# The second output product of pair 1 made whole at the end of its phase, as that of pair 2 is

## What is computed

```
x   = rms_norm(x) * rms_g
x   = (silu(x @ w_gate) * (x @ w_val)) @ w_out        # FFN 1, 1536 hidden columns
out = silu(x @ w2_in) @ w2_out                        # FFN 2, 2048 hidden columns
```

## Time and profile before

| what | value |
|---|---|
| median of 3 runs | 873.72 us (873.68 to 873.9) |
| the profiled execution, its own time | 873.36 us |
| its span, first to last instruction | 871.6 us |
| PE busy | 862.1 us, 99% |
| DVE busy | 545.3 us, 63% |
| ACT busy | 351.2 us, 40% |
| POOL busy | 413.5 us, 47% |
| DMA | 229.47 MB, mean 263 GB/s |
| granted TensorE clock | 0.5 up to 17.3 us, then 1.0 |

### The profile page before, as it was taken

The page is one execution under the profiler, slowest core; times in us unless marked ns, Lnnn a source line. Parts: engine busy times, 40 slices in busy tenths (PEclk is TensorE's granted clock), DMA queues, the critical chain, the costliest instruction groups (busy, mean ns, idle before and its releaser), DMA issues.

```text
span 871.6 us, 13511 instructions
## 1 busy us (share of the span) xinstructions
PE 862.1 (99%) x5112; PEld 830.8 (95%) x5112; DVE 545.3 (63%) x840; ACT 351.2 (40%) x648; POOL 413.5 (47%) x425
## 2 busy tenths in 40 slices
PE   7999999999999999999999999999999999999998
PEld 7999999999999999999899899999998998999998
DVE  6789757766557666655564355679676754345862
ACT  3679744542222223346553122225334332234531
POOL 6898999882347681657773000130035545203200
PEclk9999999999999999999999999999999999999999
DMA  9971678778899994656779366776768788586671
GB/s 261 280 202 32 250 276 322 276 290 316 303 332 356 348 354 152 242 199 259 267 295 372 151 236 259 275 280 254 298 239 325 266 311 290 200 311 260 242 274 73
DMA packets 79488, 229.47 MB, mean 263 GB/s; under 512 B 22720, under 2 KB 47296, under 8 KB 66752
## 3 DMA queue, kind: packets, MB, share of 16 engines
q1 hardware_dynamic: 79424, 228.61, 72.8%
HBM read 153.09 MB, written 75.50 MB: 262 GB/s over the span
## 4 chain that ended last, share of the span: by engine, by line
PE 97%; DVE 1%; DMA 1%; ACT 0%; issue 0%; SPq 0%; DVEq 0%; ACTq 0%
PE ps L1918 17%; PE ps L1920 16%; PE ps L1919 16%; PE ps L1986 5%; PE ps L1987 5%; PE ps L1985 5%; PE ps L1960 4%; PE ps L1962 4%; PE ps L1961 4%; PE ps L1847 4%; PE ps L1816 2%; PE ps L2051 2%; PE ps L2050 2%; PE ps L2049 2%; PE ps L2015 2%; PE ps L2016 2%
## 5 line engine op out<-in xcount | busy, mean ns | idle before, releaser
L1918 PE MATMUL ps<-xh,wr 128*128 128x384 f32 x840 | 282.7, 337 | 0.1
L1920 PE MATMUL ps<-xh,wr 128*128 128x384 f32 x840 | 281.3, 335 | 0.0
L1919 PE MATMUL ps<-xl,wr 128*128 128x384 f32 x840 | 281.1, 335 | 0.0
L1918 PEld LDWEIGHTS ps<-xh,wr 128*128 128x128 f32 x840 | 157.7, 188 | 3.7 <-DVE qt L1502 1.2
L1919 PEld LDWEIGHTS ps<-xl,wr 128*128 128x128 f32 x840 | 157.7, 188 | 0.6
L1920 PEld LDWEIGHTS ps<-xh,wr 128*128 128x128 f32 x840 | 157.7, 188 | 0.0
L1987 PE MATMUL ps<-wo,al 128*128 128x512 f32 x192 | 75.0, 391 | 0.0
L1986 PE MATMUL ps<-wo,ah 128*128 128x512 f32 x192 | 75.0, 390 | 0.0
L1985 PE MATMUL ps<-wo,ah 128*128 128x512 f32 x192 | 74.7, 389 | 0.0
L1521 DVE TENSOR_TENSOR qt<-ps,qt 128x384 f32<-128x384 f32 x84 | 46.0, 555 | 41.6 <-PE ps L1920 41.4
L1146 ACT ACTIVATE qt<-qt 128x384 f32<-128x384 f32 x102 | 52.5, 523 | 45.8 <-DVE qt L1521 45.3
(11 more groups left out here) (198 smaller groups left out, 1816.5 us busy)
## 6 DMA issues: line engine op xcount, KB each, us to landing
wr<-ring_home SPq DMA_DIRECT2D x40, 1792.0 KB, 8.4
ring_home<-wr SPq DMA_DIRECT2D x20, 1792.0 KB, 8.0
out_home<-wo SPq DMA_DIRECT2D x14, 1024.0 KB, 9.3
wo<-out_home SPq DMA_DIRECT2D x14, 1024.0 KB, 8.0
fw<-fold_home SPq DMA_DIRECT2D x7, 1536.0 KB, 6.7
ending_home<-eb SPq DMA_DIRECT2D x16, 512.0 KB, 6.1
ew<-ending_home SPq DMA_DIRECT2D x4, 2048.0 KB, 7.9
raw_c<-in_moe_w_out SPq DMA_DIRECT2D x13, 512.0 KB, 8.1
```

The costliest lines, as they stand in the source:

```text
L1918: pe.matmul(out_ps, w_hi, x_hi, start=first and c == 0, stop=False, skip_group_check=True)
L1919: pe.matmul(out_ps, w_hi, x_lo, start=False, stop=False, skip_group_check=True)
L1920: ins = pe.matmul(out_ps, w_lo, x_hi, start=False, stop=c == 1, skip_group_check=True)
```

## The change

Phase 4 becomes like phase 5. Its Silu columns are kept in `eh`, it has no downs, and an ending follows its last unit; the eight downs of phase 4 go. The functions of the ending get an argument e, 0 for phase 4 and 1 for phase 5. With it:

- The products of both endings come in a new order, forms 0, 1, 3, 4, 5, 6, 2 of the first factor. Products 0 and 1 share two PSUM banks in turns, so tile 2 of product 1 (i = 1, t = 2) waits for the column sum c11 of tile 0, and DVE's order at the start of an ending is rewritten.
- Low and high parts of product 0 are made in the last two units, two each.
- POOL makes weight sums c0 to c3 in phase 3, ahead of that phase's hidden sums, and c4 to c7 after the whole product; then for each ending four sums of form 3 and four of form 5. The sums have two homes in SBUF.
- Phase 5's token forms are made within the ending of phase 4, from product 3 on. Ring loads of units 52 to 54 wait for that ending (products 4 and 5), and the output of pair 1 is stored behind the ring load of unit 55.
- SP's queue has an `ending` item for each; the weights of an ending come into four homes, with product 0's load asked for at the third last unit.

```diff
-    WHOLE, ENDING = 3, 5
-
-    XHOME = [0, 1, 0, 1, 1, 0]
+    WHOLE, ENDINGS = 3, (4, 5)
+
+    XHOME = [0, 1, 0, 1, 1, 1]
...
-            pending = None if ph in (WHOLE, ENDING) else len(downs)
+            pending = None if ph >= WHOLE else len(downs)
             downs.append((ph, g))
         if ph == WHOLE:
             items.append(("whole", ph))
-    items.append(("ending", ENDING))
+        if ph in ENDINGS:
+            items.append(("ending", ph))
...
+    EPRODUCTS = [(0, 0, 0, True), (0, 1, 1, True), (2, 3, 3, True), (1, 4, 4, True), (1, 5, 5, False), (1, 2, 6, False),
+                 (2, 6, 2, False)]
...
-    ESUMS = {"u2": (0, 1), "u3": (ET, 2), "c22": (ET + 1, 2), "c11": (3 * ET, 1), "c21": (4 * ET, 1),
+    ESUMS = {"c11": (0, 1), "u2": (ET, 1), "u3": (2 * ET, 2), "c22": (2 * ET + 1, 2), "c21": (4 * ET, 1),
              "c12": (5 * ET, 1)}
...
+    EHOME = [0, 1, 2, 0, 1, 3, 0]
+    pieces = [EPART if fw < 3 else 1 for _, fw, _, _ in EPRODUCTS]
+    e_load = [[16 * sum(pieces[m] * (e + (m <= i)) for m in range(NF) if EHOME[m] == EHOME[i]) for i in range(NF)]
+              for e in range(2)]
+
+    ELOW_AT = [[], [], [], [0, 1, 2], [3, 4], [5, 6, 7], [8, 9, 10]]
+    EHIGH_AT = [[], [], [], [0], [1, 2, 3], [4, 5], [6]]
...
+    CHOME = [1, 0, 1, 0, 0, 1, 0, 1]
+    C_AT = {first_unit[(WHOLE, WHOLE + 1)[j // EPART]] + (2, 4, 6, 7, 0, 2, 3, 4)[j]: j for j in range(2 * EPART)}
...
+                if u in ending_next:
+                    sp.wait_ge(s_end, ET * (5 if u == ending_next[0] else 6))
...
+            def load_ending(e, i):
+
+                f, done = EPRODUCTS[i][1], ET * NF * e
+                if i == 0 and e == 0:
+                    sp.wait_ge(s_wh, 2 * NF)
+                    sp.wait_ge(s_cst[1], 32 * EPART)
+                    sp.wait_ge(s_cst[0], 32 * EPART)
+                elif i == 0:
+                    sp.wait_ge(s_end, done)
                 elif i < 3:
-                    sp.wait_ge(s_prod, NF * (last_unit[ENDING] + i - 1))
-                else:
-                    sp.wait_ge(s_end, ET * (i - 2))
+                    sp.wait_ge(s_prod, NF * (last_unit[ENDINGS[e]] + i - 1))
+                elif i == 5:
+
+                    sp.wait_ge(s_elo, EPART * (NF * e + 5))
+                else:
+                    sp.wait_ge(s_end, done + ET * (i - 2))
...
+                if kind == "ending":
+                    for i in range(2, NF):
+                        load_ending(ENDINGS.index(x), i)
+                    if x == ENDINGS[0]:
+                        for u in ending_next:
+                            load_ring(u)
...
-                if item == ("unit", first_unit[WHOLE + 1]):
+                if item == ("down", last_down[WHOLE - 1]):
                     load_raw(made_at["c", 0])
-                if kind == "unit" and 0 < x - first_unit[WHOLE + 1] <= 2 * EPART:
-                    keep(made_at["c", x - first_unit[WHOLE + 1] - 1])
-                if item == ("unit", first_unit[ENDING] + 2):
-                    load_ending(0)
-                if item == ("unit", last_unit[ENDING] - 1):
-                    load_ending(1)
+                if item == ("unit", first_unit[WHOLE] + 1):
+                    load_raw(made_at["c", 1])
+                if item == ("whole", WHOLE):
+                    load_raw(made_at["c", 5])
+                if kind == "unit" and x in C_AT:
+                    keep(made_at["c", C_AT[x]])
+                for e, ph in enumerate(ENDINGS):
+                    if item == ("unit", last_unit[ph] - 2):
+                        load_ending(e, 0)
+                    if item == ("unit", last_unit[ph] - 1):
+                        load_ending(e, 1)
+                if item == ("unit", first_unit[ENDINGS[1]]):
+                    sp.wait_ge(s_ec, esum(0, "c12", ET - 1))
+                    store(ENDINGS[0], range(PT))
...
+            for j in range(EPART):
+                ending_weight_sums(made_at["c", j])
             first_group = downs.index((WHOLE, 0))
             for j in range(PART):
                 hidden_sums(3, j)
             for j in range(PART):
                 hidden_sums(5, j)
-            for i in range(MADE, len(made)):
-                ending_weight_sums(i)
-            for f in (3, 5):
-                for j in range(EPART):
-                    ending_hidden_sums(f, j)
+            pool.wait_ge(s_wh, 2 * NF)
+            for j in range(EPART, 2 * EPART):
+                ending_weight_sums(made_at["c", j])
+            for e in range(2):
+                for f in (3, 5):
+                    for j in range(EPART):
+                        ending_hidden_sums(e, f, j)
...
+            def act_ending(e):
+                u = last_unit[ENDINGS[e]]
+                silu(u, 2)
+                silu(u, 3)
+                ending_high(e, 1, [EPART - 1])
                 for t in range(ET):
-                    ending_copy(t)
-                for i in range(2, NF):
-                    ending_high(i)
+                    ending_copy(e, t)
+                for i in range(1, NF):
+                    if i + 1 < NF:
+                        ending_high(e, i + 1)
+                    if e == 0:
+                        for f in EHIGH_AT[i]:
+                            token_high(ENDINGS[1], f)
...
-                if ph == ENDING and EPART - 1 <= g < 2 * EPART - 1:
-                    ending_high(0, [g - EPART + 1])
-                if x == last_unit[ENDING]:
-                    ending_high(1)
+                if ph in ENDINGS and g >= 2 * EPART - 2:
+                    i = g - 2 * EPART + 2
+                    ending_high(ENDINGS.index(ph), 0, range(2 * i, 2 * i + 2))
+                if ph in ENDINGS and x == last_unit[ph]:
+                    ending_high(ENDINGS.index(ph), 1, range(EPART - 1))
...
+            def dve_ending(e):
+                ending_low(e, 1)
+                ending_low(e, 2, (0, 1))
+                ending_sum(e, "c11", 0)
+                ending_low(e, 2, (2, 3))
+                for j in range(EPART):
+                    ending_hidden_sums(e, 4, j)
+                ending_sum(e, "c11", 1)
+                ending_sum(e, "c11", 2)
+                for i in range(2, NF):
                     if i + 1 < NF:
+                        ending_low(e, i + 1)
+                    if i == 2:
                         for j in range(EPART):
+                            ending_hidden_sums(e, 6, j)
+                    if e == 0:
+                        for k in ELOW_AT[i]:
+                            token_part(ENDINGS[1], k)
                     for t in range(ET):
                         if i == 3:
+                            ending_sum(e, "u2", t)
                         if i == 4:
+                            ending_sum(e, "u3", t)
+                            ending_sum(e, "c22", t)
                         if i == 5:
+                            ending_sum(e, "c21", t)
                         if i == 6:
+                            ending_sum(e, "c12", t)
...
-                if ph == ENDING and EPART - 1 <= g < 2 * EPART - 1:
-                    ending_low(0, [g - EPART + 1])
+                if ph in ENDINGS and g >= 2 * EPART - 2:
+                    i = g - 2 * EPART + 2
+                    ending_low(ENDINGS.index(ph), 0, range(2 * i, 2 * i + 2))
...
+            def ending(e):
+                u, snaps = last_unit[ENDINGS[e]], ET * e
+                for i, (_, _, _, first) in enumerate(EPRODUCTS):
+                    pe.wait_ge(s_ew[EHOME[i]], e_load[e][i])
                     for t in range(ET):
 
+                        if i == 0 and t == 0 and e == 0:
+                            pe.wait_ge(s_wc, 10)
+                            pe.wait_ge(s_wout, 2)
+                        elif i == 0 and t == 0:
+                            pe.wait_ge(s_ec, esum(0, "c12", ET - 1))
                         elif i == 0 and t == 2:
+                            pe.wait_ge(s_esnap, snaps + 1)
+                        elif i == 1 and t < 2:
+                            pe.wait_ge(s_esnap, snaps + 2 + t)
+                        elif i == 1:
+                            pe.wait_ge(s_ec, esum(e, "c11", 0))
+                        elif i == 2 and t == 0:
+                            pe.wait_ge(s_perm, perm0[WHOLE])
                             pe.wait_ge(s_rot, rot0[ND])
+                        elif i == 3 and t == 0:
+                            pe.wait_ge(s_silu, 4 * units[u][3] + 1)
+                            pe.wait_ge(s_c, 5 * (u + 1))
                         elif i == 4:
+                            pe.wait_ge(s_ec, esum(e, "u2", t))
                         elif i == 5:
+                            pe.wait_ge(s_ec, esum(e, "u3", t))
                         elif i == 6:
+                            pe.wait_ge(s_ec, esum(e, "c22", t))
```

(38 more changed lines are left out.)

254 lines of the change are left out of this document (112 added, 142 removed).

## The result

The changed kernel takes 875.9 us (median of 11 runs, 874.78 to 876.63), the kernel before 873.72 over its 11 runs on the same chip: a ratio of 1.0022, 95% interval 1.0013 to 1.0031. It is slower by 2.2 us. The profiled execution took 876.44 us; its span is 874.7.

What follows compares the result with a forecast made beforehand. TensorE was taken as the bound, busy 862.1 of 871.6 us. From 873.36: less 66.0, plus 60.4 (matmuls), 9.1 (port) and 0.1 (phase 3 gates) gives 876.96; with the median 0.36 above the profiled execution, 877.3; range 872.0 to 880.3.

Steps and rivals of the forecast that it cites:

- The sign and the mechanism: Slower, chance 0.72: at each ending's start VectorE and GpSimd queue for one SBUF port, and TensorE waits.
- the forecast's own range: Total time if the main forecast, chance 0.64, holds: 876.0 to 879.0 us.
- The matmuls: Phase 4 on TensorE: 66.0 us of downs and 512-column matmuls removed, 60.4 us of 504 ending matmuls added; 5.6 us gained.
- The port: Start of each ending: GpSimd's sums and VectorE's low parts take turns, TensorE 4.55 us late per ending, 9.1 for two.
- the price of one turn: At an ending's start, one GpSimd sum (1.82 us) and one VectorE low part (0.87) were taken to add up in full.
- T + 18.5: When six sums and six low parts free the port for c11; T is the start of an ending's first matmul.
- Costs put at nothing: Work beside the endings (token parts, ring loads, weight loads, pair 1's store, ScalarE's copies) was said to be covered: 0 us.
- Groups c0 to c3 in phase 3: Weight sums on GpSimd moved to phase 3, meeting V unit gates on VectorE: 0 to 0.8 us, 0.1 taken.
- the first ending's first weights: Weight loads on SyncE: a product's weights had at least 8.6 us to land in 7.9, so no cost.
- (a): Rival, chance 0.19: the port does not pile up before c11 of tile 0; faster, 869.0 to 870.0 us.
- (b): Rival, chance 0.08: GpSimd holds the port longer (6.0 per ending) or u2's 0.6 us are used up; 879.9 to 881.
- (c): Rival, chance 0.09: one ending is hit and the other half or not; 870 to 875.7 us.

Runs made afterwards that it cites:

- Experiment 6: Changed kernel with product 0's parts made in earlier units, behind c6's landing, and c4 to c7 kept at units 44 to 47: 868.51 us, ratio to before 0.9937.
- experiment 2: Changed kernel with only weight sum group c5 stored one unit earlier, at unit 45 instead of 46: 875.17 us, ratio to before 1.001.
- experiments 5: Changed kernel with product 0's parts made in earlier units, the first ending's in its sixth and seventh, behind c6's landing: 869.95 us, ratio to before 0.9951.
- experiment 3: Changed kernel with GpSimd's sixteen form 3 and 5 sums cut to 8 of 384 columns, output not the reference's: 869.51 us, ratio to before 0.9946.
- experiment 1: Changed kernel with product 0's parts made one by one in earlier units, fifth to seventh (phase 4) and fourth to seventh (phase 5): 875.44 us, ratio to before 1.0012.
- experiment 7: Kernel before with one part of the change alone, its ending's product 0 parts made two each in the last two units: 877.96 us, ratio 1.0046.

## Why the prediction was right, and where it was off

The sign and the mechanism were right: 877.3 was said, 875.9 measured, 3.6 us slower forecast and 2.2 found. The time is inside the range but 0.1 us under the forecast's own range (876.0 to 879.0). In the stage, where the cause lies, only 1.8 of the 3.6 us were found (245.0 less 243.14).

**The matmuls.** Right to a tenth. Experiment 6 has the change without waits, and its stage is 5.6 us shorter (243.14 less 237.55), the 66.0 less 60.4 of the prediction.

**The port.** In the second ending the place of all the waits was as forecast: parts 2 and 3 of product 0, part 3 of product 1, tile 2 of product 1, and none later. In the first, a wait for weights that was not forecast stood in place of the early ones. The size was off: 9.1 us for two endings, measured 245.0 less 237.55, 7.4. The term that failed is the price of one turn. I had added a sum's 1.82 and the 0.87 between two low parts, 2.69; the rows show 2.52 (the timeline of DVE above, 809.89 to 812.42). If a sum keeps the port for its 1.82, a low part keeps POOL out for about 0.70 us only. Six turns make it 1.0 us less, c11 begins at T + 17.5 and not T + 18.5, and TensorE is 3.7 us late in the second ending instead of 4.55. A row of before had shown this: the 384-wide instruction of 569.49 delayed POOL by 0.31 (2.16 for 1.85), less than it takes; I read it for the order and not for the size.

**Costs put at nothing.** The token parts, the ring loads of units 52 to 54 and the store were covered: phase 5 ran full. Groups c0 to c3 in phase 3 cost 0.05 us (81.23 for 81.18 from the start of the phase's second unit to the end of its last), 0.1 said. One cover I had not looked at: the first ending's first weights. They wait for c7, whose chain (POOL waits 6.6 and 8.4 us for the stores of groups before it, which landed in 10.6 us in the median instead of 6.1, and SP takes each group up only when a unit is done) ended 1.5 us late. The trace of experiment 2 shows that this cost nothing beside the port, experiments 5 and 6 that it is worth 1.4 us by their medians, 2.7 by their profiled executions, once the port is free. It was luck that the sum was not upset by it: the port's queue hid a term that the prediction had put at nothing.

**The rivals.** (a), no pile-up, is what experiment 3 looks like with the sums away; with them it fell. (b) fell, since the turns were strict. (c) fell, both endings were hit alike: 3.7 us in the first with the weights' wait in it, 3.7 in the second.

## What to carry to other kernels

Work handed from one engine to another in a chain is placed by its first link: making four small parts one to three units later left six 1.8 us sums of another engine behind the one boundary that had no room, where there had been two. Where two engines take turns like these, price the meeting as the sum of both queues from the moment both have work (here it was a little less, 2.52 for a pair and not 2.69), and look which result TensorE waits for at the end of it. And before moving a step earlier, look for the store or load that its memory waits for: experiment 1 won 7.4 us in the endings and lost 6.1 between two units, for a wait in one in-order queue.

## What the runs showed that I had not expected

- The queues of VectorE and GpSimd took strict turns: twelve instructions in a row, pairs 2.52 us apart, in both endings of the changed kernel. In experiment 7 POOL was again held up for 15 us. The share of a low part is about 0.70 us of its 0.87.
- A wait in one place can be free because another one is pinned to the same starting point. Removing part of the weights' wait in experiment 2 only moved it.
- Behind a gap of 4.4 us in TensorE's work the granted clock fell (0.60 over the 4 us from its end on, matmuls of 384 columns 0.32 us apart instead of 0.173), while behind each of the waits of 1.2 to 2.5 us in the endings there was no more than one slow matmul, 0.10 us.
